# First pairs of attention: the third pair's root moves to GpSimd, one pair's high halves move ahead of a square, and two row means move down in VectorE's order

## What is computed

```
q_n = q / sqrt(mean(q*q) + 1e-6) * g_q ; k_n likewise with g_k
attn = softmax(q_n @ k_n.T / 8) @ v                          # per head
x = (sigmoid(x @ w_gate) * (x @ w_val)) @ w_out              # 768 -> 1536 -> 768
e = argmax(x @ router); out = gate_w * eom * relu(x @ w1[e]) @ w2[e]    # 8 experts
```

## Time and profile before

| | |
|---|---|
| median of three runs | 1102.33 us (1100.25 to 1102.65) |
| the profiled execution | 1099.79 us |
| its span, first to last instruction | 1098.0 us |
| around the span | 1.8 us |
| TensorE busy | 1064.9 us of the span, 97% |
| VectorE, ScalarE, GpSimd busy | 555.3, 427.8 and 237.5 us |
| attention | 0 to 279 us |
| first dense layer | 279 to 770 us |
| routed layer | 770 to 1098 us |

### The profile page before, as it was taken

How to read it: one execution, slowest core, us unless ns; L and a number is a source line. 1 busy time by engine, 2 the same in 40 slices (tenths; PEclk the granted TensorE clock), 3 DMA queues, 4 the chain that set the end, 5 groups by cost and what they waited for, 6 DMA issues and landing times.

```text
span 1098.0 us, 17675 instructions
## 1 busy us (share of the span) xinstructions
PE 1064.9 (97%) x6464; PEld 558.2 (51%) x6465; DVE 555.3 (51%) x867; ACT 427.8 (39%) x613; POOL 237.5 (22%) x211
## 2 busy tenths in 40 slices
PE   7999898999999999999999999999999999999997
PEld 3443333343555555555555555556555555555554
DVE  7888777775333333333333331005574655555741
ACT  6787878787311111111111120001352542443531
POOL 4686767671000000000000100000111121112111
PEclk9999999999999999999999999999999999999999
DMA  6254756442311111111100432000573554455710
GB/s 156 63 132 120 167 143 148 118 106 52 90 58 58 58 58 57 57 57 57 57 29 1 158 101 86 29 29 30 192 265 133 213 180 175 166 188 203 276 35 18
DMA packets 117593, 118.61 MB, mean 108 GB/s; under 512 B 71600, under 2 KB 93486, under 8 KB 117536
## 3 DMA queue, kind: packets, MB, share of 16 engines
q1 hardware_dynamic: 113952, 106.37, 31.9%
q0 software_dynamic: 3168, 11.02, 3.0%
q10 hardware_dynamic: 416, 0.47, 0.2%
HBM read 99.49 MB, written 13.85 MB: 103 GB/s over the span
## 4 chain that ended last, share of the span: by engine, by line
PE 78%; POOL 12%; issue 8%; DMA 1%; ACT 1%; DVE 0%; SPq 0%; POOLq 0%; ACTq 0%; DVEq 0%
PE ps L1689 30%; PE ps L1704 15%; PE ps L1783 12%; PE ps L1761 12%; POOL arena L654 5%; POOL arena L664 3%; PE ps L1585 3%; POOL arena L650 2%; PE ps L1770 1%; PE ps L1748 1%; PE ps L1559 1%; POOL arena L647 1%; PE ps L1830 1%; DMA arena<-in_qk 1%; DMA arena<-y_parts,arena 0%
## 5 line engine op out<-in xcount | busy, mean ns | idle before, releaser
L1689 PE MATMUL ps<-arena 128*128 128x448 f16 x1728 | 328.8, 352 | 0.0
L1689 PEld LDWEIGHTS ps<-arena 128*128 128x128 f16 x1728 | 168.2, 98 | 156.1 <-issue 0.5
L1704 PE MATMUL ps<-arena 128*128 128x392 f16 (+1 forms) x996 | 165.3, 329 | 0.0
L1761 PE MATMUL ps<-arena 128*128 128x512 f16 x648 | 145.6, 379 | 0.9 <-DVE arena L1449 0.9
L1250 DVE SCALAR_TENSOR_TENSOR arena<-arena 128x768 f16<-128x768 f32 (+1 forms) x112 | 113.2, 1067 | 64.3 <-ACT arena L965 63.5
L1783 PE MATMUL ps<-arena 128*128 128x384 f16 x816 | 135.4, 326 | 0.0
L1704 PEld LDWEIGHTS ps<-arena 128*128 (+1 forms) x996 | 97.3, 98 | 66.9
L932 ACT ACTIVATE arena<-ps 128x448 f32<-128x448 f32 x48 | 26.1, 544 | 258.5 <-PE ps L1689 258.5
L1585 PE MATMUL ps<-arena 128*128 128x448 f32 x288 | 126.6, 562 | 0.0
L1106 DVE TENSOR_REDUCE arena<-ps 112x2 f16<-112x896 f32 x96 | 101.5, 1085 | 34.8 <-PE ps L1536 34.8
L1224 DVE SCALAR_TENSOR_TENSOR arena<-ps,arena 128x448 f32<-128x448 f32 x48 | 30.0, 625 | 172.1 <-PE ps L1689 92.7
(11 more groups left out here) (186 smaller groups left out, 1003.4 us busy)
## 6 DMA issues: line engine op xcount, KB each, us to landing
arena<-in_moe_w SPq DMA_DIRECT2D x48, 512.0 KB, 5.3
arena<-in_moe_w SPq DMA_DIRECT2D x64, 384.0 KB, 4.7
arena<-in_qk SPq DMA_DIRECT2D x23, 448.0 KB, 4.2
y_parts<-arena SPq DMA_DIRECT2D x16, 384.0 KB, 2.3
arena<-sums_inv SPq DMA_DIRECT2D x48, 112.0 KB, 2.8
arena<-in_v SPq DMA_DIRECT2D x24, 192.0 KB, 2.8
arena<-in_moe_w_gate SPq DMA_DIRECT2D x12, 384.0 KB, 4.3
arena<-in_moe_w_val SPq DMA_DIRECT2D x12, 384.0 KB, 5.4
```

Source lines behind the costliest of these rows:

```text
L1689: last = nc.tensor.matmul(ps[:, 2 * (b % 2) + g, 0:S], up_w[s][:, g, c, wl], xt[:, b * KC + c, xl], start=(c == 0 and wl + xl == 0), stop= ...
L1704: last = nc.tensor.matmul(ps[:, 4 + 2 * s + h, 0:cols], gt[:, f, gl, bass.ds(t * 128, 128)], wo[:, f, wl, h, 0:cols], start=(f == 0 and gl ...
L1761: last = nc.tensor.matmul(ps[:, b, :], x_t[:, xl, c], w1_s[s][:, c, wl, b * 512:(b + 1) * 512], start=(c == 0 and xl + wl == 0), stop=(c = ...
```

## The change

`first_roots(2)` and `first_inverse(2)` go. In their place GpSimd makes `inverse_rms(2)` ahead of `normalise(2)`, which now reads `rms_inv`. On ScalarE `first_roots(1)` comes in front of `high_qk(0)`, and `take_squares(2)` behind it. On VectorE `mean_squares(2)` moves from ahead of `low_q(0)` to behind `shift_rows(0)`, `first_inverse(1)` moves ahead of `low_q(0)`, and `mean_squares(3)` moves from behind `low_k(1)` to the end of the loop's first round, behind `low_k(2)`.

```diff
-                inv = first_inv[:, n] if n < 3 else rms_inv
+                inv = first_inv[:, n] if n < 2 else rms_inv
 ...
-            for n in range(3):
+            for n in range(2):
                 normalise(n)
+            inverse_rms(2)
+            normalise(2)
             for n in STEPS:
 ...
             first_roots(0)
             take_squares(1)
-            take_squares(2)
+            first_roots(1)
             act.wait_ge(gain_ready, 1)
             high_qk(0)
-            first_roots(1)
-            first_roots(2)
+            take_squares(2)
             nc.scalar.activation(tables[:, 1:2], rms_eps, ACT.Exp).then_inc(tables_ready, 1)
             take_squares(3)
             high_qk(1)
 ...
             mean_squares(1)
             dve.wait_ge(eye_loaded, 16)
             nc.vector.tensor_copy(ident, cst[:, 0:128]).then_inc(ident_ready, 1)
-            mean_squares(2)
+            first_inverse(1)
             low_q(0)
             dve.wait_ge(scratch_ready, 3)
             maxima(0, 0)
-            first_inverse(1)
-            first_inverse(2)
             maxima(0, 1)
             maxima(0, 2)
             maxima(0, 3)
             low_k(0)
             dve.wait_ge(const_loaded, 16)
             shift_rows(0)
+            mean_squares(2)
             low_q(1)
             low_k(1)
-            mean_squares(3)
             for n in range(3):
 ...
                 shift_rows(n + 1)
                 low_q(n + 2)
                 low_k(n + 2)
+                if n == 0:
+                    mean_squares(3)
             v_low(2)
```

More of the change, by code:

```diff
@@ L158, in attention_moe_moe_kernel @@
         neg_max = [at2.take(PT, 128, F16).rearrange("p (h m) -> p h m", h=2) for _ in range(2)]
-        first_rms = at2.take(PT, 3 * 2 * HJ, F32).rearrange("p (n c) -> p n c", n=3)
-        first_inv = at2.take(PT, 3 * 2 * HJ, F32).rearrange("p (n c) -> p n c", n=3)
+        first_rms = at2.take(PT, 2 * 2 * HJ, F32).rearrange("p (n c) -> p n c", n=2)
+        first_inv = at2.take(PT, 2 * 2 * HJ, F32).rearrange("p (n c) -> p n c", n=2)
         rms_eps = at2.take(PT, 1, F32)
```

## The result

The changed kernel takes 1111.55 us in the median of four runs (1109.27 to 1112.15), the kernel before 1102.43 us (1100.25 to 1102.65; a fourth run of 1102.54 us has joined the three given above). The ratio is 1.0083, 95% interval 1.0064 to 1.0103: slower by 9.1 us. The profiled execution took 1109.27 us, with a span of 1107.5. The forecast was 1109.5 us in a range of 1106.8 to 1112.5.

The account below looks back on a forecast made before the run. The prediction took TensorE, busy for 97% of the span, to bound the kernel. A 6.75 us stall plus 1.5 us for the clock gave 8.25 us on a level of 1101.3: 1109.5 us, range 1106.8 to 1112.5.

Parts of the forecast that it names:

- The stall: TensorE ahead of weigh_end(0): the late mean of pair 3 delays end_low(0) on GpSimd, start 33.28 instead of 26.53, +6.75 us.
- One of its signs: TensorE idle for over 7 us ahead of line 1576, released by line 688.
- The price of the root on GpSimd: Pair 2 normalised at 22.78 instead of 17.38, its transposes near 22.87, a lead of 0.30; costs nothing against before.
- The bounds for the stall: weigh_end(0) late by +7.05 us if every earlier lead is lost, +5.64 if leads are kept whole down to low_k(2).
- The clock: TensorE behind weigh_end(0): idle time drops the clock from 2.4 to 1.2 GHz, and coming back adds 1.5 us.
- the sign: Granted clock 0.5 for some 3 us around 29 to 36, first matmuls of lines 1576 and 1585 twice as far apart.
- My upper end of 3.4: Most the clock's recovery behind weigh_end(0) could cost, in us: twice the start's price, if it stays down longer.
- rival (a): Stall at weigh_end(0) without a clock cost, TensorE keeping or regaining its clock at once: 6.75 alone, 1108.1 us; chance 0.12.
- rival (b): Stall at weigh_end(0) plus a longer stretch at 1.2 GHz, up to 3.4 us: 1111.5 us; chance 0.10.
- The sum: Delay at weigh_end(0) plus clock recovery, 6.75 + 1.5 = 8.25 us, carried through the later stages to the end.
- Rival (c): Later attention absorbs the delay in 12.1 us of TensorE waits for line 845's exponentials: 1101.0 us; chance 0.04.
- Rival (d): end_low(0) on GpSimd isn't held, pair 3's mean costs nothing, early leads count 0.3 to 1.4 us: 1100 to 1101; chance 0.02.

Follow-up runs that it names:

- the kernel before, mended: Kernel before with end_low(n) ahead of inverse_rms(n + 3) on GpSimd for three first pairs and mean_squares(3) behind v_low(0) on VectorE: 1101.06 us, ratio 1.0002.
- only the root: Kernel before with only pair 2's root moved to GpSimd, both means left in place: 1102.96 us, ratio 1.0012.
- only the high halves: Kernel before with only ScalarE's order changed, high_qk(0) and first_roots(1) ahead of take_squares(2): 1103.25 us, ratio 1.0022.

## Why the prediction was right

**The stall.** The prediction had `weigh_end(0)` at 33.28; with the 0.69 of the late load that is 33.97, and 34.01 was measured. +6.75 forecast, +6.79 measured. Each step of the chain held within 0.16 us: the first maximum at 11.96 - 0.69 = 11.27 (11.11 forecast; the high halves started 0.10 behind the transposes, not 0.04), pair 2's transposes at 23.62 - 0.69 = 22.93 with GpSimd as releaser (22.87), pair 3's mean at 26.45 - 0.69 = 25.76 (25.70), `end_low(0)` done at 33.91 - 0.69 = 33.22 (33.20). It could be so close because every link of it was a row of the same kind in the trace before, and none had to be guessed. One of its signs didn't come as written: the profile names "issue" and not line 688 as what ended the wait, and the cause shows only in GpSimd's rows and in the run with `end_low(0)` first.

**The price of the root on GpSimd.** "The cover is just enough, and this part costs nothing against before" held for pair 2's transposes. But it was too short a look: the run with pair 3's mean put back shows that the same chain holds `end_low(0)` for 2.70 us once pair 3 follows at once. In the changed kernel the later mean hid that cost completely. The bounds for the stall didn't name it. The sum wasn't touched by it, because GpSimd was free at 23.57 and pair 3's mean came only at 27.66.

**The clock.** This term was mis-sized: 1.5 forecast, 2.33 in the profile and 1.49 to 2.34 over the kernels that stalled. I had taken the price of the first 20 matmuls of the program from one trace, 1.7 us. Behind the stall TensorE worked for 5.4 us at the lower clock, from 34.01 to about 39.4, where the sign named "some 3 us around 29 to 36". The one start was a poor measure: over the twelve traces the first 20 matmuls take from 5.87 to 7.13 us, which puts the same price between 1.6 and 2.9. My upper end of 3.4 held. The rows from 29 to 40 us show the clock's fall and its price; so rival (a), a stall without it, is out for the profile. By the Trainium skill's rule ("TensorE: Matmul & The Clock Gate", section "HAM oscillation"), each gap which throttles is paid for anew; the one gap of this trace agrees, with 2.33 us behind it. The size lies nearly half way to rival (b)'s end.

**The sum.** 6.79 + 2.33 = 9.12 us, and the medians differ by 9.12; the forecast had 8.25. That the two agree to the hundredth is luck: the profiled executions differ by 9.50, and the rest of attention alone took 236.1 us in this trace and 239.0 in the next one of the same kernel. The forecast of 1109.5 us is lower than the measured 1111.55 by 0.9 for this sum and by 1.1 for the level, since I had weighed the low profiled execution into it (1101.3), and the median of before is 1102.43. Both misses go the same way, and the range was wide enough for their sum.

**Rival (c)**, the stall absorbed in the later waits for the exponentials, is out: attention's last `weigh_end` is 10.11 us later, 9.42 without the late load. These waits still come to 12.2 us, where they were 12.1; they moved along with TensorE. **Rival (d)**, `end_low(0)` not held, is out by GpSimd's rows (line 688 comes behind pair 3's line 664), and the run with `end_low(0)` first shows that this place in the queue is what counts.

## What to carry to other kernels

Before an instruction is moved down on one engine, follow its signal: whatever stands behind the instruction that waits for it, on the other engine, is moved down too. Here a row sum whose pair TensorE doesn't need until 33.25 us (pair 3's transposes in the kernel before) fed a GpSimd queue in which a short, urgent subtraction stood last, and that subtraction was 0.15 us from being critical although the profile named another engine as releaser. Put the urgent short ones first in a queue that runs in order: here that took the stall from 6.79 to 0.69 us.

A stall of TensorE costs more than its length where its clock falls: 7.7 us cost another 2.0 to 2.3, 3.5 us another 1.5, and 1.6 us nothing in the profiled execution. Its length alone doesn't decide, as the next section shows.

## What the runs showed of the hardware

The same work at the same place doesn't always pay the same for the clock. Behind the stalls it came back after 5.4, 4.7 and 5.5 us of work (7.7 us of idle time, three traces) and after 3.2 us (3.5 us of idle time). At the program's start the first 20 matmuls take from 5.87 to 7.13 us. The kernel before and the kernel before, mended:

```profile
1.13 6.01 PE L1502 MATMUL ps<-arena 128*128 128x512 f16 x20 [1.13 <-DVE arena L1030]
```

```profile
1.13 7.13 PE L1503 MATMUL ps<-arena 128*128 128x512 f16 x20 [1.13 <-DVE arena L1030]
```

The column of the granted clock doesn't show this: it reads 1.00 from the start on, also where the kernel before's weight loads start 0.42 us apart (1.96, 2.38) and not 0.21. That the clock is low there is inferred from this rate. What sets the length can't be told from these runs.

The clock also fell in the middle of attention, in four of the twelve traces (`end_low(0)` first, only the root, only the high halves, before with the mend), each time at or shortly behind a wait of 1.95 to 2.26 us for the exponentials. In the mended kernel before:

```profile
112.25 1.30 PE L1560 MATMUL ps<-arena 64*64 64x448 f16 x6 [2.13 <-ACT arena L845]
```

```profile
113.00:114.00 1.00, 1.00 (x8) 0.30 (x6) 0.00 (x0) 0.27 (x2) 1.00 (x2) 0.50 0.99 341
```

It was low for about 3.4 us, and TensorE is busy for 221.9 to 222.1 us between the second and the last `weigh_end` of these four, 220.3 to 220.7 in the other eight: 1.6 us, as much as the effects that the small experiments were after. The kernel before and the changed one have waits of up to 2.13 us in front of the same line without a fall, so the length of one wait doesn't decide it.

The rest of the scatter can't be laid to differences between kernels either. From the second `weigh_end` to the last the traces go from 235.8 to 239.9 us, and the changed kernel alone has 236.1 and 239.0. Of these 2.9 us, 2.1 lie in TensorE's waits for the maxima of line 1107 (1.8 us in the one, 3.9 in the other); why they grow isn't shown.
